# Second MLP of a three-stage kernel: u = 1 + z moves from GpSimd to ScalarE

## The reference, cut to what matters

```python
def _moe2_ref(x, w_in, w_out):
    h = x @ w_in                                           # 2304x512 @ 512x2048
    g = np.maximum(h, 0.0) + np.log1p(np.exp(-np.abs(h)))  # softplus
    return (g @ w_out).astype(np.float32)                  # 2304x2048 @ 2048x512
```

## Time and profile before

| | us |
|---|---|
| median of 3 runs | 910.83 (910.66 to 911.72) |
| the profiled execution, its own time | 911.15 |
| its span, first to last instruction | 909.4 |
| PE busy | 869.7 (96%) |
| DVE busy | 762.1 (84%) |
| ACT busy | 501.7 (55%) |
| POOL busy | 433.4 (48%) |
| mean granted TensorE clock | 0.994 of 2.4 GHz |

### The profile page before, as it was taken

One profiled execution on the slowest core, in us unless ns is written; L12 is line 12 of the kernel. 1 busy time (PEld: TensorE's weight loads), 2 busy tenths in 40 slices (PEclk: granted clock), 3 DMA queues, 4 the chain that ended last, 5 costly groups with the idle time before them and its releaser, 6 DMA issues.

```text
span 909.4 us, 16546 instructions
## 1 busy us (share of the span) xinstructions
PE 869.7 (96%) x6104; PEld 726.3 (80%) x6104; DVE 762.1 (84%) x1376; ACT 501.7 (55%) x936; POOL 433.4 (48%) x449
## 2 busy tenths in 40 slices
PE   6899999999989999999998998999999999999997
PEld 4566666666667889889898897999989999899995
DVE  6999999999929754835641999999999999999997
ACT  4777877888846442433442564545545455455543
POOL 3445444447617612313311565565555556556563
PEclk9999999999999999999999899999999999999999
DMA  6813431342100000000002610000000000000000
GB/s 163 217 32 80 102 97 37 80 105 75 48 25 23 24 1 1 1 1 1 1 12 88 197 30 0 36 1 1 35 1 1 35 1 1 35 0 0 35 0 35
DMA packets 29496, 37.65 MB, mean 41 GB/s; under 512 B 3696, under 2 KB 17520, under 8 KB 29424
## 3 DMA queue, kind: packets, MB, share of 16 engines
q1 hardware_dynamic: 29024, 36.42, 14.5%
q10 hardware_dynamic: 400, 0.30, 0.1%
HBM read 31.98 MB, written 4.72 MB: 40 GB/s over the span
## 4 chain that ended last, share of the span: by engine, by line
DVE 53%; PE 35%; issue 8%; POOL 1%; ACT 1%; DMA 0%; ACTq 0%; DVEq 0%; POOLq 0%
DVE g L850 12%; PE y_ps L1044 11%; DVE ntop L710 8%; PE s_ps L942 7%; DVE g_hi L854 7%; DVE g L840 5%; PE h_ps L911 5%; DVE g_lo L856 5%; DVE g L843 5%; PE o_ps L982 4%; PE f_ps L1101 3%; PE m_ps L1020 2%; DVE x_lo L705 2%; DVE solu L807 1%; DVE st_top L793 1%
## 5 line engine op out<-in xcount | busy, mean ns | idle before, releaser
L451 POOL TENSOR_TENSOR w_lo<-w_raw,w_hi 128x512 fp32r<-128x512 f32 x96 | 129.6, 1351 | 163.6 <-ACT w_hi L632 163.6
L412 POOL TENSOR_SCALAR kept<-kept,inv 128x576 f32<-128x576 f32 x144 | 106.1, 756 | 117.9 <-DVE inv L742 117.8
L511 ACT ACTIVATE expd<-s_ps,ntop 128x576 f32<-128x576 f32 x144 | 106.3, 741 | 51.7 <-DVE ntop L710 51.7
L1020 PE MATMUL m_ps<-y_hi,w_lo 128*128 128x384 f32 x384 | 131.4, 342 | 0.0
L648 ACT ACTIVATE l<-u 128x384 f32<-128x384 f32 x96 | 50.4, 525 | 145.8 <-POOL u L459 145.8
L1020 PE MATMUL m_ps<-y_lo,w_hi 128*128 128x384 f32 x384 | 130.3, 339 | 0.0
L1020 PE MATMUL m_ps<-y_hi,w_hi 128*128 128x384 f32 x384 | 129.2, 336 | 0.0
L459 POOL TENSOR_TENSOR u<-z,consts 128x384 f32<-128x384 f32 x96 | 108.2, 1127 | 41.8 <-ACT z L641 41.7
L850 DVE TENSOR_TENSOR g<-g,l 128x384 f32<-128x384 f32 x96 | 125.7, 1309 | 2.7
L1101 PE MATMUL f_ps<-w_hi,g_hi 128*128 128x512 f32 x288 | 115.4, 401 | 8.9 <-DVE g_lo L856 8.9
L710 DVE TENSOR_REDUCE ntop<-s_ps 128x1 f32<-128x576 f32 x144 | 107.5, 757 | 14.2 <-PE s_ps L942 6.8
(11 more groups left out here) (87 smaller groups left out, 1815.1 us busy)
## 6 DMA issues: line engine op xcount, KB each, us to landing
q_sb<-q_t SPq DMA_DIRECT2D x28, 288.0 KB, 5.1
v_sb<-v_main SPq DMA_DIRECT2D x16, 256.0 KB, 3.2
stage<-w_in SPq DMA_DIRECT2D x16, 256.0 KB, 2.7
w_raw<-w_out SPq DMA_DIRECT2D x8, 512.0 KB, 4.8
out<-o_sb SPq DMA_DIRECT2D x5, 768.0 KB, 3.5
k_sb<-k_t SPq DMA_DIRECT2D x21, 144.0 KB, 4.4
stage<-w_in SPq DMA_DIRECT2D x4, 512.0 KB, 8.9
stage<-w_out SPq DMA_DIRECT2D x4, 512.0 KB, 3.7
```

Source lines behind the costliest of these rows:

```text
L412: nc.gpsimd.tensor_scalar(kept[:, tile % RING, :], kept[:, tile % RING, :], inv[:, group % 2, k:k + 1], 1.0, ALU.mult, ALU.mult).then_inc( ...
L451: nc.gpsimd.tensor_tensor(w4[1][:, n % 2, :], w4_raw[:, n % F2, :], f32(w4[0][:, n % 2, :]), ALU.subtract).then_inc(w4lo_made, 1)
L511: nc.scalar.activation(expd[:, tile % 2, :].rearrange("p (a b) -> p a b", a=2), s_ps[tile % 2][:, :, 0:HALF], ACT.Exp, bias=ntop[:, tile % ...
L1020: last = nc.tensor.matmul(m_ps[n % 4][:, 0:GC], w[:, k, (n % F2) * P:(n % F2 + 1) * P], y[odd][:, k, :], start=(k == 0 and m == 0), stop=( ...
```

## The change

`one_plus` goes from the GpSimd program to the ScalarE program. There it is an activation, `Identity` with a bias of 1.0 from a column of constants, between the exponential and the logarithm of the same item. It waits for the exponential and for the logarithm of item j-2, no longer for L840 of item j-2 (for which the item's |h| waits already). GpSimd's loop has `w4_low` alone. ScalarE waits once for the constants. In the last two items ScalarE runs soft(94), soft(95), `w4_high(94)`, `w4_high(95)`. VectorE's, TensorE's and SyncE's programs are the same.

```diff
@@ GpSimd
-            def one_plus(j, n):
-                pool.wait_ge(z2_made, j + 1)
-                wait(pool, l2_made, j - 1)
-                wait(pool, t2_made, j - 1)
-                nc.gpsimd.tensor_tensor(u2[:, n % 2, :], z2[:, n % 2, :], consts[:, 3:4].broadcast_to([P, GC]),
-                                        ALU.add).then_inc(u2_made, 1)
             for j in range(2 * F2):
-                one_plus(j, j)
                 w4_low(j, j)
-            with pool.Fori(1, MG // 2 - 1) as i:
+            with pool.Fori(1, MG // 2) as i:
                 for n in range(2 * F2):
-                    one_plus(2 * F2 * i + n, n)
                     w4_low(2 * F2 * i + n, n)
...
-            for n in (2 * F2 - 2, 2 * F2 - 1):
-                one_plus(last + n, n)
-            for n in (2 * F2 - 2, 2 * F2 - 1):
-                w4_low(last + n, n)
@@ ScalarE
+            act.wait_ge(ones_made, 6)
...
+            def one_plus(j, n):
+                slot = n % 2
+                act.wait_ge(z2_made, j + 1)
+
+                wait(act, l2_made, j - 1)
+                nc.scalar.activation(u2[:, slot, :], z2[:, slot, :], ACT.Identity, bias=consts[:, 3:4]
+                                     ).then_inc(u2_made, 1)
...
             def soft(j, n):
                 exponential(j, n)
+                one_plus(j, n)
                 logarithm(j, n)
...
             soft(last + n, n)
-            exponential(last + n + 1, n + 1)
+            soft(last + n + 1, n + 1)
             w4_high(last + n, n)
-            logarithm(last + n + 1, n + 1)
             w4_high(last + n + 1, n + 1)
```

More of the change, by code:

```diff
@@ L452, in w4_low @@
                                         ALU.subtract).then_inc(w4lo_made, 1)
-            def one_plus(j, n):
-                pool.wait_ge(z2_made, j + 1)
-                wait(pool, l2_made, j - 1)
-                wait(pool, t2_made, j - 1)
-                nc.gpsimd.tensor_tensor(u2[:, n % 2, :], z2[:, n % 2, :], consts[:, 3:4].broadcast_to([P, GC]),
-                                        ALU.add).then_inc(u2_made, 1)
             for j in range(2 * F2):
-                one_plus(j, j)
                 w4_low(j, j)
-            with pool.Fori(1, MG // 2 - 1) as i:
+            with pool.Fori(1, MG // 2) as i:
                 for n in range(2 * F2):
-                    one_plus(2 * F2 * i + n, n)
                     w4_low(2 * F2 * i + n, n)
-            last = F2 * (MG - 2)
-            for n in range(2 * F2 - 2):
-                one_plus(last + n, n)
-                w4_low(last + n, n)
-            for n in (2 * F2 - 2, 2 * F2 - 1):
-                one_plus(last + n, n)
-            for n in (2 * F2 - 2, 2 * F2 - 1):
-                w4_low(last + n, n)
         @block.scalar
```

## The result

The kernel after takes 901.93 us (median of 6 runs, 901.80 to 904.17) against 910.21 for the kernel before on the same chip (6 runs, 907.11 to 911.72): a ratio of 0.9917, 95% interval 0.9900 to 0.9933. The forecast was 902.5. The profiled execution took 901.92 us for a span of 900.2, against 909.4 before.

The account below looks back on a forecast made before the run. PE was taken to set the pace at 4.21 us an item, leaving only its gaps: 2.0 + 4.0 + 2.3 = 8.3 us off 911.15, with the median 0.32 lower, 902.5 us. Range 899.5 to 907.2.

Parts of the forecast that it names:

- What bounds the kernel: Second MLP: PE sets the pace at 4.21 us an item; only its gaps, 13.6 us together, can be won.
- A: First item of the second MLP: PE's 3.62 us wait and slow clock behind it; gain 2.0 us (0.3 to 4.8).
- B: Item 13, behind a new group's input low part: PE's wait and slow clock go, 4.0 us (0 to 4.0).
- C: Last two items: PE's 2.57 us wait and 0.55 us more; forecast gain 2.3 us (1.0 to 3.1).
- ScalarE gains u at no cost: Each item: u takes 0.60 us on ACT, which stays under PE's 4.21 us pace, so it costs nothing.
- rival 4: Identity missing from the loaded table set: two loads of 1.28 us in each item, about 1016 us; chance 0.02.
- GpSimd gives back DVE's time: Without u on GpSimd, DVE gains 0.5 us an item: 3.75 us in items 0 to 11, under 3.7 later.
- Rival 1: Ports stay the limit: DVE at PE's pace in items 0 to 11, B stays; 906.4 to 907.7 us, chance 0.19.
- The clock: Behind A's wait: 1.2 of the 2.87 us lost to the slow clock come back (0 to 2.87).
- 6 us of backlog: Items before B: 0.5 us an item over 12 items gives 6 us of slack, perhaps 3.5 kept, against 2.36 needed.
- The sum: Whole kernel: A 2.0, B 4.0 and C 2.3 make 8.3 us, for a median of 902.5 us.

Follow-up runs that it names:

- e4: The kernel after, with a GpSimd addition of the same shape, its result used by nobody, in u's old place: 910.82 us, ratio 1.0012.
- e7: The kernel after, with the two parts of the last two weight blocks made four to six items earlier, in free input buffers: 900.95 us, ratio 0.9904.
- e5: The kernel before, with 24 transposes of the identity into an unused PSUM bank in TensorE's wait at A: 912.41 us, ratio 1.0020.
- e2: The kernel before, with u made by ScalarE in items 12 to 15 alone: 907.72 us, ratio 0.9979.
- e1: The kernel before, with u made by ScalarE in items 0 to 11 alone: 904.43 us, ratio 0.9936.
- e3: The kernel before, with u on ScalarE in the last two items alone, in the order of the kernel after: 907.80 us, ratio 0.9971.
- e12: e11 with 12 transposes of the identity in TensorE's wait at A: 899.08 us, ratio 0.9869 against the kernel before.
- e11: The kernel after, with the changes of e7 and e8 in one: 900.64 us, ratio 0.9878.
- e8: The kernel after, with all blocks of w_in split before the second MLP begins: 901.65 us, ratio 0.9898.

## Why the prediction was right, step by step

**What bounds the kernel.** Right: PE at 4.2 us an item in the middle, the gain only at A, B and C. The three gaps carry all of the 9.2 us.

**ScalarE gains u at no cost.** Right: 0.60 us forecast, 618 ns measured. The one table load is still the only one, so rival 4 is void:

```profile
L468 ACT ACT_TABLE_LOAD x1 | 1.3, 1283 | 4.3 <-issue 4.3
```

**GpSimd gives back DVE's time.** Right in kind, shown by e4, and the relief was put much too low in the middle: I allowed just under 3.7 us an item, the window gives 34.00 / 50 x 4.2 = 2.86. Once DVE has slack it does most of its work while POOL waits. In items 0 to 11 the relief was put too high: 3.75 us forecast, but the low parts of g come every 4.28 us from item 1 to item 10 (504.25 to 542.76), and DVE is busy 43.89 of 45 us. This is the step that failed, "With 3.75 us an item DVE is no longer behind, and the same 2.85 us find 0.5 x 12 = 6 us of slack". The slack in items 2 to 9 is 0.6 to 0.7 us and does not grow. Rival 1 had the pace right, and was wrong that B would stay.

Busy for 43.89 of 45 us does not mean that DVE has 4.2 us of work there; it has 3.2 (2.6 and 0.6 for the low part of w_in). One instruction an item is held until w_lo ends, and w_lo comes every 4.20 us, since the high part before it (L614) waits for PE's matmuls. From the kernel after, between items 4 and 5:

```profile
515.15 0.62 ACT L614 CAST w_hi<-w_raw 128x512 fp32r<-128x512 f32 x1 [0.91 <-PE f_ps L1091]
...
515.85 1.63 POOL L451 TENSOR_TENSOR w_lo<-w_raw,w_hi 128x512 fp32r<-128x512 f32 x1 [2.59 <-ACT w_hi L614]
...
516.25 1.65 DVE L830 SCALAR_TENSOR_TENSOR g<-u,z 128x384 f32<-128x384 f32 x1
```

So here PE sets DVE's pace, by way of ScalarE and GpSimd, and the slack hardly moves. In e7, with the same instructions in these items but 1.36 us of slack at item 1, w_lo meets the low part of w_in instead, and the slack stays at 2.06 us from item 3 to item 11:

```profile
516.57 1.76 DVE L782 TENSOR_TENSOR w_lo<-stage,w_hi 128x512 fp32r<-128x512 f32 x1
```

**A.** The start at 499.95 came at 499.85, with the working as laid out, L451 against the cast of g:

```profile
494.95 0.62 ACT L630 ACTIVATE u<-z,consts 128x384 f32<-128x384 f32 x1
...
497.26 0.55 DVE L840 TENSOR_TENSOR g<-g,l 128x384 f32<-128x384 f32 x1
...
497.51 1.43 POOL L451 TENSOR_TENSOR w_lo<-w_raw,w_hi 128x512 fp32r<-128x512 f32 x1 [36.46 <-ACT w_hi L614]
...
497.85 1.31 DVE L844 CAST g_hi<-g 128x384 fp32r<-128x384 f32 x1
```

The cast L844 started 0.34 us behind L451 and took 1.31 us, where it takes 0.36 unhindered. The Trainium skill (SBUF — State Buffer, section "SBUF: two separate sides") says that whichever of two such instructions starts first keeps the shared ports for its whole length, and this row agrees. The 499.95 had L451 hold DVE in that way; how long a whole item takes does not follow from it, and there I went wrong (above).

The clock was a term of 1.2 us, and 2.6 came between items 0 and 1, since in this execution the clock stayed at 1.00 behind the wait of 2.72 us; in four of six executions the mean clock is 1.00 (901.80 to 901.94 us), in two 0.996 (903.94, 904.17). The forecast had taken the slow clock of a shorter wait, and none came, so this term was 1.4 us too small and right in its sign alone. Not all of it was kept: e5 shows that full clock at A is worth nothing while DVE can't follow; the change gives DVE just enough to follow (at item 1 the slack is 0.06 us, so PE all but waits) and pays 0.8 us back by item 12. What the clock itself is worth here can be read from e7, which has the same instructions in these items and lost it: item 0 to item 12 takes 52.02 us there, 51.46 in the kernel after and 53.29 before. So of the 1.8 us won on this stretch the clock accounts for 0.6, measured against the fall in e7 (0.66 from 500 to 505 us, where before has 0.51).

**B.** It went, as forecast, 4.2 us against 4.0. The way was another. Let s be the slack at item 12 and d the time from the end of its low part of g to the end of item 13's, the next input's low part between them; item 13 is on time if s + 4.2 - d is above zero. From the timelines:

| | s | d | s + 4.2 - d | PE's wait |
|---|---|---|---|---|
| before | 0.80 | 7.48 | -2.48 | 2.36 |
| e2, u on ACT in 12 to 15 | 1.46 | 6.39 | -0.73 | 0.64 |
| e1, u on ACT in 0 to 11 | 2.59 | 6.05 | 0.74 | none |
| after | 2.40 | 5.42 | 1.18 | none |

Both terms moved, and not 6 us of backlog. d is read here, first in the kernel before, then in the kernel after:

```profile
552.70 0.56 DVE L856 TENSOR_TENSOR g_lo<-g,g_hi 128x384 fp32r<-128x384 f32 x1
...
559.68 1.06 DVE L856 TENSOR_TENSOR g_lo<-g,g_hi 128x384 fp32r<-128x384 f32 x1
```

```profile
548.35 0.56 DVE L846 TENSOR_TENSOR g_lo<-g,g_hi 128x384 fp32r<-128x384 f32 x1
548.83 1.75 DVE L772 TENSOR_TENSOR y_lo<-xt,y_hi 128x1536 fp32r<-128x1536 f32 x1
550.50 1.66 DVE L830 SCALAR_TENSOR_TENSOR g<-u,z 128x384 f32<-128x384 f32 x1
...
553.77 0.56 DVE L846 TENSOR_TENSOR g_lo<-g,g_hi 128x384 fp32r<-128x384 f32 x1
```

The next input's low part takes 1.75 us where it took 2.85: I had carried its hindered length over. The instruction behind it is still held once, 1.66 us, by w_lo.

**C.** 2.3 us forecast, 2.25 measured. Item 95 started 2.29 us behind item 94, between the 2.2 and 2.8 us of the two orders that were worked out; what was left was L451, as said, and e7 took it away for 1.0 us. That part of C needs DVE relieved before item 94 as well (e3) was not in the working.

**The sum.** 8.3 us forecast. Between the medians of one chip it is 910.21 - 901.93 = 8.3; between the two profiled executions it is 9.2, since the one of before (911.15) lies 0.9 above that chip's median. Of the terms, A was 1.5 too low, the 0.8 lost in items 2 to 12 was not in the sum, and B and C were within 0.2. That the difference of the medians agrees with the forecast to a tenth is luck: the 1.5 and the 0.8 partly cancel, the 0.9 between the two ways of comparing takes up the rest, and the slack that carried B came another way.

## What to carry to other kernels

When two engines share a path to memory, ask of an instruction moved off one of them not what it cost there but what it held up; adding it back as a dummy with no data in common (e4) settles it in one run. An engine that is always busy need not be full: if what holds it is released by the engine that it feeds, it runs at that engine's pace, and less work alone may not show in its busy time. A slow clock, or a gap, on the engine that sets the pace is only worth its time if the next engine has slack: measure the slack of each item before repairing it (with the same trick e5 lost 0.2%, and e12 took away the slower executions of e11). An instruction's length read in a crowded stretch is not its length; a chain of spare microseconds worked out from it can be right in sum and wrong in each term.

## What the runs showed of the hardware

- The granted clock fell to the 1.2 GHz level for a part of the 5 us from 500 to 505 us behind a PE wait of 1.95 us (e8, mean 0.66). Behind one of 2.72 us the mean over the same 5 us was 1.00 in the kernel after and 0.66 in e1 and e7. Behind C's 2.57 us before, the nine matmuls ran at full pace. The length of the wait alone doesn't tell. With the wait filled but for 0.63 us (e12) the mean clock was 0.999 or 1.00 in all four executions.
- What a GpSimd instruction costs DVE is not in proportion to its length. The five instructions of a DVE item take 2.59 us unhindered (0.55 + 0.56 + 0.56 + 0.36 + 0.56). Their means from 600 to 840 us add up to 2.79 us beside w_lo alone (the kernel after), and to 3.90 us beside w_lo and a second addition of 1.12 us, whether that is u (before) or nobody's (e4, 3.89). The 1.37 us of w_lo cost 0.2 us an item, the next 1.12 us cost 1.1. In items 0 to 11 of the kernel after, where DVE has 0.6 us more of its own, w_lo alone costs it about 1 us an item (4.28 less 3.2), since there it holds up a DVE instruction in every item; in the middle, in 10 of the 16 items of a group, it runs while DVE waits for ACT and overlaps DVE's work by 0.1 us or less.
